# The experts' second product with tokens in the rows: 9 products of 512 columns for 12 of 384, shares applied to the outputs, and PE transposing the sum for the last stage

## The chip, the cores and the metric

One core of one Trainium2 chip. The metric is the device time of one execution in microseconds, median of several runs. PE is TensorE, DVE is VectorE, ACT is ScalarE, POOL is GpSimd, SP is the engine that issues most of the DMA transfers.

## What is computed

Three stages, one after the other on N = 1152 tokens of width 512:

```
x = banded attention(q, k, v)                       # 2 batches, 8 heads of 64, window 64
p = probs / sum(probs)                              # [N, 4], "the shares"
for e in 4 experts:                                 # F = 1024 hidden
    h = max(x @ w1[e], 0)
    out += p[:, e] * (h @ w2[e])
h = out @ w_in;  g = h * cos(h);  result = g @ w_out    # 2048 hidden, run as two halves of 1024
```

## The kernel before

Every float32 product on PE is made of three products of rounded parts: high by high, high by low, low by high (names `x_hi`, `x_lo`, `w_hi`, `w_lo`, `hp_hi`, `hp_lo`). The four experts and the two halves of the last layer are six blocks of 1024 hidden units. A block goes over three groups of TOK = 384 tokens; one group of one block is a **turn**, and a turn has FC = 8 **steps**, one for each 128 hidden units. So there are 12 expert turns (numbers 0 to 11) and 6 turns of the last layer, and 96 expert steps.

A step on PE is an up product and a down product. `up` makes 128 hidden units x 384 tokens, 12 matmuls of 384 columns (4 pieces of the input width, 3 parts each). `down` adds the step's hidden units to the turn's output. PE runs up three steps ahead of down (LAG = 3), so the order is up(s+3), down(s), up(s+4), down(s+1).

Between the two, in an expert step: DVE takes the up product out of its PSUM bank with max(.,0) times the share (`weigh`, L654; the shares lie broadcast over all partitions in `p_bc`), ACT rounds it to `hp_hi` (L493), and DVE subtracts to get `hp_lo` (L648). In the last layer ACT and DVE compute the cosine in its place (L498, L681, L683, L686, L505, L507, L694).

In an expert step the down product is laid out with output width in the rows: for each of 4 pieces of width, `w` is the stationary operand and the hidden units of 384 tokens stream through (L879: 4 x 3 matmuls of 384 columns, into the 4 banks `y_ps`). The sum `acc` is therefore width x tokens, the layout that the last layer's up product reads as its input. In the last layer the down product has the tokens in the rows: for each of 3 pieces of 128 tokens the hidden units are stationary and 512 columns of `w_out` stream (L882: 3 x 3 matmuls of 512 columns, 3 banks). At the end of a turn DVE adds the banks to `acc` (`take_outputs`, L673 and L675). After the last expert POOL rounds and subtracts `acc` into `x_hi` and `x_lo` (`next_input`, L428 and L430).

The first expert's first turn is woven into the attention: in each of its 8 steps PE has, besides up and down, the transposes of attention weights (`transpose_probs`, L827), the attention outputs (`outputs`, L843) and the scores of a later unit (`scores`, L807). The down product is cut in two there, in front of `outputs` and behind it. DVE takes the row maxima of the scores (L614) and copies the first transposed half out of PSUM (`copy_first`, L629), ACT the second half.

The order on each engine is written out by hand and kept by semaphores. The shares come in by one DMA of 72 rows of 256 bytes (L448), DVE divides (L597 to L603), and they go to a scratch area in DRAM and back by broadcasting DMAs into `p_bc`.

Of the kernel before, what the change touches and what calls it, by code (L numbers as in the profile page):

```python
# [17 lines left out]
P = 128  # L18
# [19 lines left out]
OC = TOK // P  # L38
HALVES = F2 // F1
TURN = NTOK * FC  # L40
LAG = 3
BLOCKS = E + HALVES

# [45 lines left out]
def build(nc, q, k, v, probs, weights, out):  # L89
    with ExitStack() as ctx:  # L90
# [11 lines left out]
        p_bc = sb("p_bc", [P, E, N])  # L102
# [39 lines left out]
        JP = 16  # L142
        dp_raw = part(JP, E)
        dp_sum = part(JP)
        dp_inv = part(JP)
        dp_out = part(E, JP)
# [20 lines left out]
        p_scratch = nc.dram_tensor("p_scratch", [E, N], F32, kind="Internal").ap()  # L167
# [22 lines left out]
        dp_in, dp_done, dp_stored = sem("dp_in"), sem("dp_done"), sem("dp_stored")  # L190
        p_first_tile_in, p_first_in, p_in = sem("p_first_tile_in"), sem("p_first_in"), sem("p_in")
# [13 lines left out]
        h_taken = sem("h_taken")  # L205
# [3 lines left out]
        y_taken = sem("y_taken")  # L209
        x2_hi_done = sem("x2_hi_done")  # L210
# [6 lines left out]
        C_H, C_HI, C_DOWN, C_Y = HB, HP, HP, DC  # L217
# [3 lines left out]
        def y_count(turn, c):  # L221
            if isinstance(turn, int) and turn >= MIX:
                return MIX * DC + (turn - MIX) * OC + c + 1 + C_Y
            return turn * DC + c + 1 + C_Y
# [13 lines left out]
        def _(sp):  # L238
# [36 lines left out]
            for f in range(FIRST):  # L275
# [3 lines left out]
            sp.wait_ge(dp_done, 4)  # L279
            sp.dma_start(p_scratch.rearrange("e (p j) -> p e j", j=JP),  # L280
                         dp_out[0:N // JP, :, :]).then_inc(dp_stored, 16)
# [6 lines left out]
            sp.wait_ge(dp_stored, 16)  # L288
            sp.dma_start(p_bc[:, 0, 0:TOK], p_scratch[0:1, 0:TOK].to_broadcast([P, TOK])).then_inc(p_first_tile_in, 16)
# [15 lines left out]
            sp.dma_start(p_bc[:, 0, TOK:N], p_scratch[0:1, TOK:N].to_broadcast([P, N - TOK])).then_inc(p_first_in, 16)  # L305
            load_v(8)
            load_qk(11)
            for e in range(1, E):
                load_v(8 + e)
                sp.dma_start(p_bc[:, e, :], p_scratch[e:e + 1, :].to_broadcast([P, N])).then_inc(p_in, 16)  # L310
# [18 lines left out]
        def _(pool):  # L329
# [92 lines left out]
            def next_input(t):  # L422

                pool.wait_ge(y_taken, y_count((E - 1) * NTOK + t, DC - 1))
                for c in range(DC):
                    cell = acc[:, t, c * TOK:(c + 1) * TOK]
                    at = slice(t * TOK, (t + 1) * TOK)
                    nc.gpsimd.tensor_copy(x_hi[:, c, at], cell).then_inc(x2_hi_done, 1)  # L428
                    pool.wait_ge(x2_hi_done, t * DC + c + 1)
                    last = nc.gpsimd.tensor_tensor(x_lo[:, c, at], cell, x_hi[:, c, at], ALU.subtract)  # L430
                last.then_inc(x2_lo_done, 1)

# [3 lines left out]
            for t in range(NTOK - 1):  # L436
                next_input(t)
            for f in range(FC):
                low_weights(f, E * FC + f, COS_PART)
            next_input(NTOK - 1)  # L440
# [5 lines left out]
        def _(act):  # L446
            act.sem_inc(hp_hi_done, C_HI)
            act.dma_start(dp_raw[0:N // JP, :, :],  # L448
                          probs.rearrange("(p j) e -> p j e", j=JP)).then_inc(dp_in, 16)
# [40 lines left out]
            def hidden_high(f, s):  # L490
                act.wait_ge(h_taken, s + 1 + C_H)
                act.wait_ge(down_done, s - HP + 1 + C_DOWN)
                nc.scalar.activation(hp_hi[:, f % HP, :], h_raw[:, f % HP, :], ACT.Copy).then_inc(hp_hi_done, 1)  # L493

            def cosine(f, s, late, refill=None):
# [4 lines left out]
                if late:  # L500
                    hidden_high((f - 1) % FC, s - 1)
# [7 lines left out]
            def act_turn(e, t, turn, mix_now, mix_next, last=False):  # L509
                refills = isinstance(t, int) and t == NTOK - 1 and not last  # L510
                for f in range(FC):
                    g, s = (f + LAG) % FC, turn * FC + f + LAG
                    if last and f >= FC - LAG:
                        if f == FC - LAG:
                            hidden_high(FC - 1, s - 1)
                        continue

                    refill = (f - 1, e + 1) if refills and f > 0 else None
                    if mix_now if f < FC - LAG else mix_next:
                        hidden_high(g, s)  # L520
                        if refill is not None:
                            high_weights(*refill)
                    else:
                        cosine(g, s, not (isinstance(s, int) and s == MIX * FC), refill)
                if refills:
                    high_weights(FC - 1, e + 1)
# [22 lines left out]
            for f in range(FC):  # L549
# [3 lines left out]
                if f == 0:  # L553
                    hidden_high(0, 0)
                    copy_second(m)
                    hidden_high(1, 1)
                    hidden_high(2, 2)
                    hidden_high(3, 3)
                    exponentials(m + 2, 0)
                else:  # L560
                    if f <= FIRST:
                        hidden_high(f + FIRST - 1, f + FIRST - 1)
                    elif f > FIRST + 1:
                        hidden_high((f - 1 + LAG) % FC, f - 1 + LAG)
# [8 lines left out]
            hidden_high((FC - 1 + LAG) % FC, FC - 1 + LAG)  # L573
# [9 lines left out]
            for e in range(E - 1, BLOCKS):  # L583
                with act.Fori(0, NTOK - 1) as t:
                    act_turn(e, t, e * NTOK + t, e < E, e < E)
                act_turn(e, NTOK - 1, e * NTOK + NTOK - 1, e < E, False, last=e == BLOCKS - 1)


        @block.vector
        def _(dve):  # L590
            dve.sem_inc(h_taken, C_H)
            dve.sem_inc(y_taken, C_Y)

            def shares():
                dve.wait_ge(dp_in, 16)
                rows = slice(0, N // JP)
                nc.vector.tensor_reduce(dp_sum[rows, :], dp_raw[rows, :, :], axis=AX.X, op=ALU.add).then_inc(dp_done, 1)  # L597
                dve.wait_ge(dp_done, 1)
                nc.vector.tensor_scalar_add(dp_sum[rows, :], dp_sum[rows, :], EPS).then_inc(dp_done, 1)
# [442 lines left out]
```

## Time and profile before

| | |
|---|---|
| median of 3 runs | 651.83 us (651.81 to 651.86) |
| profiled execution | 651.55 us, of which the recorded span is 649.8 us |
| PE busy | 640.1 us, 99% |
| DVE, ACT, POOL busy | 48%, 36%, 29% |

The span runs from the first to the last recorded instruction; 1.75 us of the execution's time lie outside it. The chain of work that ended last is the list of instructions that, followed back from the end, each waited for the one before; what isn't on it had time to spare. Busy time of PE is modelled from pipelined matmuls which overlap, so the distance between the starts of two matmuls, not their duration, is what one costs.

### The profile page before, as it was taken

What the parts mean: (1) busy time and instruction counts of PE and PEld (TensorE: products, weight loads), DVE (VectorE), ACT (ScalarE), POOL (GpSimd) and SP (SyncE); (2) the same over time, 40 slices, a digit from 0 to 9 for tenths busy, and PEclk for the clock granted to TensorE, in tenths of its full rate; (3) what the DMA queues carried; (4) which work ended last, traced back from release to release, by engine and by line L of the source; (5) the groups of instructions that cost most, each with busy time, mean ns of one, the idle gap of its engine ahead of it and who ended that gap; (6) DMA issues with size and microseconds to landing.
All of it is one profiled execution on the core that took longest, in us unless ns stands there. A gap on an engine that the chain in (4) does not pass through costs nothing.

```text
span 649.8 us, 11012 instructions
## 1 busy us (share of the span) xinstructions
PE 640.1 (99%) x3980; PEld 610.1 (94%) x3980; DVE 311.8 (48%) x725; ACT 234.8 (36%) x505; POOL 185.2 (29%) x246
## 2 busy tenths in 40 slices
PE   7899999999999999999999999999999999999998
PEld 6788899999999999999999999999999999999996
DVE  6676442324232324232324242325766676756664
ACT  6685411133111133111133111137455467544452
POOL 6683200154000055000056012098800059400000
PEclk8999999999999999999999999999999999999999
DMA  8858300044000034000024100023200003001011
GB/s 277 284 166 253 127 2 0 2 130 130 1 0 0 0 100 149 10 0 0 0 93 123 46 0 0 0 66 104 92 2 1 0 33 98 0 2 48 0 49 48
DMA packets 21829, 39.59 MB, mean 61 GB/s; under 512 B 2080, under 2 KB 13472, under 8 KB 21792
## 3 DMA queue, kind: packets, MB, share of 16 engines
q1 hardware_dynamic: 21708, 39.08, 18.5%
q8 instruction: 23, 0.38, 0.2%
q14 instruction: 14, 0.11, 0.1%
q10 hardware_dynamic: 84, 0.02, 0.0%
HBM read 36.72 MB, written 2.38 MB: 60 GB/s over the span
## 4 chain that ended last, share of the span: by engine, by line
PE 96%; DVE 2%; issue 1%; ACT 1%; POOL 0%; DVEq 0%
PE bank L851 45%; PE bank L879 31%; PE bank L882 15%; PE bank L843 2%; PE bank L807 1%; PE bank L827 1%; DVE arena L614 1%; PE bank L917 1%; ACT arena L457 0%; DVE arena L629 0%; DVE arena L675 0%; DVE hp_lo L648 0%; ACT x_hi L470 0%; POOL arena L389 0%; DVE arena L634 0%
## 5 line engine op out<-in xcount | busy, mean ns | idle before, releaser
L363 POOL TENSOR_TENSOR w_lo<-w_raw,w_hi 128x128 fp32r<-128x128 f32 (+2 forms) x180 | 140.5, 812 | 287.5 <-ACT w_hi L488 286.0
L851 PE MATMUL bank<-x_hi,w_hi 128*128 128x384 f32 (+1 forms) x576 | 195.0, 339 | 0.0
L851 PE MATMUL bank<-x_hi,w_lo 128*128 128x384 f32 (+1 forms) x576 | 193.2, 335 | 0.0
L851 PE MATMUL bank<-x_lo,w_hi 128*128 128x384 f32 (+1 forms) x576 | 192.8, 335 | 0.0
L493 ACT ACTIVATE hp_hi<-h_raw 128x384 fp32r<-128x384 f32 x144 | 75.3, 523 | 287.4 <-DVE h_raw L654 283.0
L654 DVE SCALAR_TENSOR_TENSOR h_raw<-bank,p_bc 128x384 f32<-128x384 f32 x96 | 53.4, 557 | 175.8 <-PE bank L851 175.0
L879 PE MATMUL bank<-hp_hi,w_hi 128*128 128x384 f32 x384 | 129.7, 338 | 0.0
L879 PE MATMUL bank<-hp_hi,w_lo 128*128 128x384 f32 x384 | 128.4, 334 | 0.0
L879 PE MATMUL bank<-hp_lo,w_hi 128*128 128x384 f32 x384 | 128.3, 334 | 0.0
L648 DVE TENSOR_TENSOR hp_lo<-h_raw,hp_hi 128x384 fp32r<-128x384 f32 x144 | 89.4, 621 | 53.7 <-ACT hp_hi L493 53.5
L851 PEld LDWEIGHTS bank<-x_hi,w_hi 128*128 128x128 f32 x576 | 108.1, 188 | 3.4 <-issue 1.0
L851 PEld LDWEIGHTS bank<-x_lo,w_hi 128*128 128x128 f32 x576 | 108.2, 188 | 1.9
L851 PEld LDWEIGHTS bank<-x_hi,w_lo 128*128 128x128 f32 x576 | 108.1, 188 | 0.0
L879 PEld LDWEIGHTS bank<-hp_hi,w_hi 128*128 128x128 f32 x384 | 72.1, 188 | 0.5
L879 PEld LDWEIGHTS bank<-hp_lo,w_hi 128*128 128x128 f32 x384 | 72.1, 188 | 0.0
L879 PEld LDWEIGHTS bank<-hp_hi,w_lo 128*128 128x128 f32 x384 | 72.0, 188 | 0.0
L882 PE MATMUL bank<-w_lo,hp_hi 128*128 128x512 f32 x144 | 56.9, 395 | 0.0
L882 PE MATMUL bank<-w_hi,hp_lo 128*128 128x512 f32 x144 | 56.8, 395 | 0.0
L882 PE MATMUL bank<-w_hi,hp_hi 128*128 128x512 f32 x144 | 56.0, 389 | 0.0
L505 ACT ACTIVATE arena<-arena 128x384 f32<-128x384 f32 x48 | 25.2, 525 | 48.1 <-DVE arena L686 48.1
L694 DVE TENSOR_TENSOR h_raw<-arena,bank 128x384 f32<-128x384 f32 x48 | 26.5, 552 | 32.5 <-ACT arena L507 32.5
L488 ACT ACTIVATE w_hi<-w_raw 128x1024 fp32r<-128x1024 f32 x40 | 41.9, 1047 | 0.1
(55 smaller groups left out, 471.4 us busy)
## 6 DMA issues: line engine op xcount, KB each, us to landing
w_raw<-in_weights SPq DMA_DIRECT2D x43, 512.0 KB, 3.5
arena<-in_q SPq DMA_DIRECT2D x12, 192.0 KB, 4.5
result<-arena SPq DMA_DIRECT2D x9, 256.0 KB, 2.1
w_raw<-in_weights SPq DMA_DIRECT2D x8, 256.0 KB, 6.3
arena<-in_k SPq DMA_DIRECT2D x8, 224.0 KB, 5.7
p_bc<-p_scratch SPq DMA_DIRECT2D x3, 576.0 KB, 5.5
arena<-in_v SPq DMA_DIRECT2D x4, 384.0 KB, 5.9
arena<-in_v SPq DMA_DIRECT2D x4, 320.0 KB, 6.4
```

The lines of the kernel that those rows point to most:

```text
L363: last = nc.gpsimd.tensor_tensor(w_lo[:, f, at:at + part], raw[:, at - begin:at - begin + part], w_hi[:, f, at:at + part], ALU.subtract)
L488: nc.scalar.activation(w_hi[:, f, :], w_raw[:, f % STAGE, :], ACT.Copy).then_inc(w_hi_done, 1)
L493: nc.scalar.activation(hp_hi[:, f % HP, :], h_raw[:, f % HP, :], ACT.Copy).then_inc(hp_hi_done, 1)
L505: nc.scalar.activation(c_abs, c_r2, ACT.Abs).then_inc(cos_abs, 1)
L614: last = nc.vector.tensor_tensor_reduce(out=s_sb[:, g % SR, t, :], in0=s_banks(m)[h][:, chunk(t)], in1=mask[:, MASK_OF[m // PAIRS][t], :], ...
L648: nc.vector.tensor_tensor(hp_lo[:, f % HP, :], h_raw[:, f % HP, :], hp_hi[:, f % HP, :], ALU.subtract).then_inc(hp_lo_done, 1)
L654: nc.vector.scalar_tensor_tensor(out=h_raw[:, f % HP, :].unsqueeze(1), in0=ps[:, 0:TOK].unsqueeze(1), scalar=0.0, in1=p_bc[:, ds1(e), toke ...
L694: nc.vector.tensor_tensor(h_raw[:, f % HP, :], c_cos, bank_h, ALU.mult).then_inc(h_taken, 1)
L843: last = nc.tensor.matmul(o_bank(m)[heads, block_of * WIN:(block_of + 1) * WIN], v_w[:, r, WINDOW_OF[t][block_of], heads], prob_t[:, h, bl ...
L851: last = nc.tensor.matmul(ps[:, 0:TOK], w[:, f, chunk(c)], x[:, c, token_cols(t)], start=c == 0 and i == 0, stop=c == DC - 1 and i == 2)
L879: product = nc.tensor.matmul(y_ps[c][:, 0:TOK], w[:, f, DM + c * P:DM + (c + 1) * P], h[:, f % HP, :], **flags)
L882: product = nc.tensor.matmul(y_ps[c][:, :], h[:, f % HP, chunk(c)], w[:, f, DM:2 * DM], **flags)
```

## The change

- `down` has the tokens in the rows in all six blocks: 3 pieces x 3 parts of 512 columns. The fourth bank, `y_ps[3]`, is free of it.
- The shares are kept with the tokens on the partitions (`p_tok`, 128 x 4 x 9), loaded by a DMA whose runs are 4 numbers (16 bytes) long, 1152 of them. The scratch area, `p_bc` and their DMAs are gone. DVE multiplies when it adds a turn's outputs (`take_shared`).
- `weigh` is gone. ACT makes `hp_hi` from the PSUM bank with Relu, and DVE makes `hp_lo` from the same bank as max(.,0) minus `hp_hi` in one instruction; the bank is free only then. In the first turn the up products alternate between two banks (`h_bank`).
- `acc` now has tokens in the rows, so PE transposes it in 9 groups of 4 transposes of 128 x 128 (`turn_input`), one behind each of steps 3, 4 and 5 of turns 10, 11 and 12; ACT rounds (`next_input_high`) and DVE subtracts (`next_input_low`) from `y_ps[3]`. POOL has no part in it.

```diff
-            def weigh(f, s, e, t, ps):
-                dve.wait_ge(up_done, s + 1)
-                nc.vector.scalar_tensor_tensor(out=h_raw[:, f % HP, :].unsqueeze(1), in0=ps[:, 0:TOK].unsqueeze(1),
-                                               scalar=0.0, in1=p_bc[:, ds1(e), token_cols(t)],
-                                               op0=ALU.max, op1=ALU.mult).then_inc(h_taken, 1)
+            def hidden_high(f, s, ps):
+                act.wait_ge(up_done, s + 1)
+                act.wait_ge(down_done, s - HP + 1 + C_DOWN)
+                nc.scalar.activation(hp_hi[:, f % HP, :], ps[:, 0:TOK], ACT.Relu).then_inc(hp_hi_done, 1)
+            def hidden_low(f, s, ps):
+                dve.wait_ge(hp_hi_done, s + 1 + C_HI)
+                nc.vector.scalar_tensor_tensor(out=hp_lo[:, f % HP, :], in0=ps[:, 0:TOK], scalar=0.0,
+                                               in1=hp_hi[:, f % HP, :], op0=ALU.max,
+                                               op1=ALU.subtract).then_inc(hp_lo_done, 1)
...
-                        if mix:
-                            product = nc.tensor.matmul(y_ps[c][:, 0:TOK], w[:, f, DM + c * P:DM + (c + 1) * P],
-                                                       h[:, f % HP, :], **flags)
-                        else:
-                            product = nc.tensor.matmul(y_ps[c][:, :], h[:, f % HP, chunk(c)], w[:, f, DM:2 * DM],
-                                                       **flags)
+                        product = nc.tensor.matmul(y_ps[c][:, :], h[:, f % HP, chunk(c)], w[:, f, DM:2 * DM],
+                                                   start=f == 0 and i == 0, stop=f == FC - 1 and i == 2)
...
+            def take_shared(e, turn, t):
+                nc.vector.tensor_copy(p_now[:, :].unsqueeze(1),
+                                      p_tok[:, ds1(e), bass.ds(t * OC, OC)]).then_inc(p_picked, 1)
+                dve.wait_ge(p_picked, turn + 1)
+                dve.wait_ge(down_done, turn * FC + FC + C_DOWN)
+                for c in range(OC):
+                    cell = acc[:, ds1(t), c * DM:(c + 1) * DM]
...
+                        nc.vector.scalar_tensor_tensor(out=cell, in0=y_ps[c][:, :].unsqueeze(1),
+                                                       scalar=p_now[:, c:c + 1], in1=cell, op0=ALU.mult,
+                                                       op1=ALU.add).then_inc(y_taken, 1)
...
+            def turn_input(k):
+                pe.wait_ge(y_taken, y_count(MIX - NTOK + k // OC, k % OC))
+                if k > 0:
+                    pe.wait_ge(x2_lo_done, k)
+                for c in range(DC):
+                    at = k % OC * DM + c * P
+                    last = nc.tensor.transpose(y_ps[3][:, chunk(c)], acc[:, k // OC, at:at + P], ident[:, :])
+                last.then_inc(x2_turned, 1)
...
-                down_cells(f, True, (0, 1), 0)
+                down_cells(f, (0,), 0)
...
-                    down_cells(f, True, (2, 3), 0).then_inc(down_done, 1)
+                    down_cells(f, (1, 2), 0).then_inc(down_done, 1)
...
-            act.dma_start(dp_raw[0:N // JP, :, :],
-                          probs.rearrange("(p j) e -> p j e", j=JP)).then_inc(dp_in, 16)
+            act.dma_start(dp_raw, probs.rearrange("(k p) e -> p k e", p=P)).then_inc(dp_in, 16)
```

On PE, a down product inside an expert turn, before (L879 is `down_cells`, L851 the up product behind it):

```order
1451 L879 MATMUL bank<-hp_hi,w_hi 128x384 [waits hp_lo_done]
1452 L879 MATMUL bank<-hp_lo,w_hi 128x384
1453 L879 MATMUL bank<-hp_hi,w_lo 128x384
1454 L879 MATMUL bank<-hp_hi,w_hi 128x384
1455 L879 MATMUL bank<-hp_lo,w_hi 128x384
1456 L879 MATMUL bank<-hp_hi,w_lo 128x384
1457 L879 MATMUL bank<-hp_hi,w_hi 128x384
1458 L879 MATMUL bank<-hp_lo,w_hi 128x384
1459 L879 MATMUL bank<-hp_hi,w_lo 128x384
1460 L879 MATMUL bank<-hp_hi,w_hi 128x384
1461 L879 MATMUL bank<-hp_lo,w_hi 128x384
1462 L879 MATMUL bank<-hp_hi,w_lo 128x384
```

The down product at such a place after the change, in one of the nine steps that have transposes behind them (L892 is `down_cells`, L911 `turn_input`, L865 the up product):

```order
1456 L892 MATMUL bank<-w_hi,hp_hi 128x512 [waits hp_lo_done]
1457 L892 MATMUL bank<-w_hi,hp_lo 128x512
1458 L892 MATMUL bank<-w_lo,hp_hi 128x512
1459 L892 MATMUL bank<-w_hi,hp_hi 128x512
1460 L892 MATMUL bank<-w_hi,hp_lo 128x512
1461 L892 MATMUL bank<-w_lo,hp_hi 128x512
1462 L892 MATMUL bank<-w_hi,hp_hi 128x512
1463 L892 MATMUL bank<-w_hi,hp_lo 128x512
1464 L892 MATMUL bank<-w_lo,hp_hi 128x512
1465 L911 MATMUL bank<-ident,arena 128x128 [waits x2_lo_done,y_taken]
1466 L911 MATMUL bank<-ident,arena 128x128 x3
1467 L865 MATMUL bank<-x_hi,w_hi 128x384 [waits hp_lo_done,w_lo_done]
```

Twelve matmuls of 384 columns became nine of 512, and four transposes stand ahead of the next up product.

On DVE, in the second step of the woven turn, behind the last of six maxima (`arena` holds the attention's tiles; the ISA rows are the maxima), before:

```order
148 L614 ISA arena<-bank,mask 128x128
149 L614 ISA arena 128x1
150 L648 TENSOR_TENSOR hp_lo<-h_raw,hp_hi 128x384 [waits hp_hi_done]
151 L629 COPY arena<-bank 128x384 [waits p_transposed]
152 L623 TENSOR_SCALAR arena<-arena 128x3 [waits exped]
153 L625 RECIPROCAL arena<-arena 128x3 [waits summed]
154 L623 TENSOR_SCALAR arena<-arena 128x3 [waits exped]
155 L625 RECIPROCAL arena<-arena 128x3 [waits summed]
156 L654 SCALAR_TENSOR_TENSOR h_raw<-bank,p_bc 128x384 [waits hp_hi_done,up_done,hp_lo_done]
157 L643 TENSOR_TENSOR x_lo<-bank,x_hi 128x384 [waits x_hi_done]
```

The same place after:

```order
141 L613 ISA arena<-bank,mask 128x128
142 L613 ISA arena 128x1
143 L647 SCALAR_TENSOR_TENSOR hp_lo<-bank,hp_hi 128x384 [waits hp_hi_done]
144 L628 COPY arena<-bank 128x384 [waits p_transposed]
145 L622 TENSOR_SCALAR arena<-arena 128x3 [waits exped]
146 L624 RECIPROCAL arena<-arena 128x3 [waits summed]
147 L622 TENSOR_SCALAR arena<-arena 128x3 [waits exped]
148 L624 RECIPROCAL arena<-arena 128x3 [waits summed]
149 L642 TENSOR_TENSOR x_lo<-bank,x_hi 128x384 [waits x_hi_done]
```

The subtraction now reads PSUM and one SBUF tile, and `weigh` is gone from behind it.

## Rows read from the trace of the kernel before

**Rows 1.** The page: busy time of PE and the clock granted to it, in 40 slices.

```profile
PE 640.1 (99%) x3980; PEld 610.1 (94%) x3980; DVE 311.8 (48%) x725; ACT 234.8 (36%) x505; POOL 185.2 (29%) x246
...
PEclk8999999999999999999999999999999999999999
```

**Rows 2.** Groups of instructions, by form: busy us, mean ns | idle before.

```profile
L879 PE MATMUL bank<-hp_hi,w_hi 128*128 128x384 f32 x384 | 129.7, 338 | 0.0
...
L882 PE MATMUL bank<-w_hi,hp_lo 128*128 128x512 f32 x144 | 56.8, 395 | 0.0
```

**Rows 3.** The chain in order of time: start us, us, what.

```profile
88.07 2.08 PE bank L879 x12
...
449.99 2.08 PE bank L879 x12
452.07 2.08 PE bank L851 x12
454.15 2.08 PE bank L882 x9
456.23 2.10 PE bank L851 x12
...
634.17 2.08 PE bank L882 x9
```

**Rows 4.** DVE in order of time, first cosine step: start us, us, instruction.

```profile
442.23 0.65 DVE L681 TENSOR_SCALAR arena<-arena 128x384 f32<-128x384 f32 x1 [2.88 <-ACT arena L498]
```

**Rows 5.** PE in order of time, the woven turn.

```profile
73.83 0.33 PE L851 MATMUL bank<-x_hi,w_hi 128*128 128x384 f32 x1
...
74.87 0.49 PE L827 MATMUL bank<-ident,arena 128*128 128x128 f32 x3
...
76.24 0.49 PE L827 MATMUL bank<-ident,arena 128*128 128x128 f32 x3
```

**Rows 6.** Groups by form: copies, subtractions, additions and PE's old transposes.

```profile
L648 DVE TENSOR_TENSOR hp_lo<-h_raw,hp_hi 128x384 fp32r<-128x384 f32 x144 | 89.4, 621 | 53.7 <-ACT hp_hi L493 53.5
...
L827 PE MATMUL bank<-ident,arena 128*128 128x128 f32 x72 | 12.5, 287 | 2.7 <-DVE arena L629 1.9 <-POOL arena L389 0.8
...
L478 ACT ACTIVATE w_hi<-w_raw 128x512 fp32r<-128x512 f32 x4 | 2.5, 620 | 0.0
...
L675 DVE TENSOR_TENSOR arena<-bank,arena 128x512 f32<-128x512 f32 x3 | 2.0, 691 | 1.8 <-PE bank L882 1.8
```

**Rows 7.** One cosine step in order of time, PE, ACT and DVE.

```profile
562.67 0.33 PE L851 MATMUL bank<-x_hi,w_lo 128*128 x1
...
565.69 0.62 ACT L507 ACTIVATE arena<-arena,half_pi 128x384 f32<-128x384 f32 x1
...
566.43 0.56 DVE L694 TENSOR_TENSOR h_raw<-arena,bank 128x384 f32<-128x384 f32 x1 [0.86 <-ACT arena L507]
```

**Rows 8.** The chain in order of time, the woven turn.

```profile
41.98 0.94 DVE hp_lo L648
...
49.46 0.87 DVE hp_lo L648
```

**Rows 9.** PE in order of time, two places in the woven turn.

```profile
43.54 0.52 PE L827 MATMUL bank<-ident,arena 128*128 128x128 f32 x3 [0.33 <-DVE arena L629]
...
63.61 0.34 PE L879 MATMUL bank<-hp_hi,w_lo 128*128 128x384 f32 x1
63.99 0.89 PE L807 MATMUL bank<-arena 64*64 64x128 f32 x24
```

**Rows 10.** The first 7 us in order of time, DVE and PE.

```profile
3.04 0.22 DVE L597 TENSOR_REDUCE arena<-arena 72x16 f32<-72x64 f32 x1 [1.85 <-DMA arena<-in_probs]
...
3.81 0.28 DVE L603 TENSOR_TENSOR arena<-arena 72x64 f32<-72x64 f32 x1
...
6.04 0.29 DVE L614 CUSTOM_DVE_ANT_0 arena<-bank,mask 128x128 f32<-128x128 f32 x1 [1.96 <-PE bank L807]
...
6.26 0.89 PE L807 MATMUL bank<-arena 64*64 64x128 f32 x24 [0.41 <-DMA arena<-in_k]
```

More of the change, by code:

```diff
@@ L141, in build @@
         row_inv = part(PR, CT)
[L142 to L146, printed above, removed]
+        dp_raw = part(TILES, E)
+        dp_sum = part(TILES)
+        dp_inv = part(TILES)
         bank = [ctx.enter_context(nc.psum_tensor(f"bank{i}", [P, 512], F32)) for i in range(8)]
@@ L165, in o_bank, with h_bank @@
             return bank[0] if m < AHEAD else pt_ps
-        p_scratch = nc.dram_tensor("p_scratch", [E, N], F32, kind="Internal").ap()
+        def h_bank(s):
+            if s < FIRST:
+                return y_ps[s]
+            return y_ps[3] if s % 2 else bank[0]
         ident_done = sem("ident_done")
@@ L420, in _ @@
                     low_second(i + 2)
[L422 to L431, printed above, removed]
             with pool.Fori(1, E) as e:
@@ L658, in share, with next_input_low @@
-            def share(f, s, e, t):
-                weigh(f, s, e, t, h_ps[f % HB])
-                hidden_low(f, s)
-            def take_outputs(e, turn, t, mix, last=False):
-                if isinstance(e, int) and e == E:
-                    dve.wait_ge(x2_lo_done, t + 1)
+            def next_input_low(k):
+                dve.wait_ge(x2_hi_done, k + 1)
+                cell = (slice(None), slice(None), slice(k * P, (k + 1) * P))
+                nc.vector.tensor_tensor(x_lo[cell], y_ps[3][:, :].rearrange("p (c n) -> p c n", c=DC), x_hi[cell],
+                                        ALU.subtract).then_inc(x2_lo_done, 1)
@@ L665, in take_outputs @@
+            def take_outputs(e, turn, t, last=False):
+                if e == E:
+                    dve.wait_ge(x2_lo_done, (t + 1) * OC)
                 if not last:
                     dve.wait_ge(down_done, turn * FC + FC + C_DOWN)
[L667 removed]
+                for c in range(OC):
                     if last:
                         dve.wait_ge(result_done, c + 1)
[L670 to L675 removed]
@@ L677, in times_cosine @@
-            def times_cosine(f, s, late, take=None):
+                    cell = acc[:, ds1(t), c * DM:(c + 1) * DM]
+                    if e == E:
+                        nc.vector.tensor_copy(cell, y_ps[c][:, :].unsqueeze(1)).then_inc(y_taken, 1)
+                    else:
+                        nc.vector.tensor_tensor(cell, y_ps[c][:, :].unsqueeze(1), cell, ALU.add).then_inc(y_taken, 1)
+            def times_cosine(f, s, late, take=None, which=()):
                 n = s - MIX * FC
```

249 lines of the change are left out of this document (121 added, 128 removed).

## The prediction

> **What bounds the kernel now.** I read the page's busy times and granted clock first. PE is busy 99% of the span and holds 0.9 or more of its clock in every slice but the first [rows 1]: this is the upper of its two levels, 2.4 GHz. Then the chain that ended last, in order of time: from the down product at 88.07 us to the end it is PE and nothing else, in pieces of 2.08 or 2.10 us that follow each other without a gap [rows 3]. So behind 88 us only PE's own work counts, and what DVE, ACT, POOL or the DMAs are spared there is worth nothing. Ahead of 88 us, where the attention is woven in, DVE stands in the chain, and there a shorter DVE can pay.
>
> **The change, part by part.**
>
> *The down product itself.* The groups of instructions tempt to a large gain: a 384-column matmul has a mean of 338 ns, a 512-column one 395 ns [rows 2], so 12 of the one against 9 of the other would be 4.06 against 3.56 us, 0.50 us a step, 48 us over 96 steps. But these are durations of overlapping instructions. The chain gives what they cost back to back: 12 of 384 columns take 2.08 us, 9 of 512 also 2.08 us [rows 3]. Both stream 4608 columns, 173 and 231 ns a matmul, 0.451 ns a column either way. I take 0 us.
>
> The Trainium skill, "TensorE: Matmul & The Clock Gate", section "Wait — 56ns, not 53.3ns?", speaks for a small gain here: it gives a fixed 2.5 ns for each warm matmul on top of its columns. By it, three matmuls less in each of 96 steps would save an estimated 0.7 us. The row disagrees: what 384 columns take above 160 ns (384 over 2.4 GHz) is 13 ns, and 512 above 213 ns it is 18 ns, so the excess grows with the columns and nothing of it is fixed.
>
> *The pair of up and down.* One thing does differ. Between the 384-column downs at 88.07 and 449.99 lie 87 steps, 361.92 / 87 = 4.160 us a step. Between the 512-column downs at 454.15 and 634.17 lie 43 steps, 180.02 / 43 = 4.187 us [rows 3]. The up product behind a 512-column down takes 2.10 us, not 2.08. It isn't the cosine work that does it: that begins on DVE at 442.23 [rows 4], and the up product at 452.07 still takes 2.08 [rows 3]; the first slow one, at 456.23, is the first behind a 512-column down. So each step of turns 1 to 11, 88 of them, becomes 0.027 us longer: **+2.35 us**. Bounds: 0 if it were something else of the last layer, 2.6 if the 8 woven steps have it too.
>
> *The transposes.* 36 of 128 columns, all new on PE, where nothing can hide them. In the woven turn, 12 up matmuls with one group of 3 transposes among them take 76.24 − 73.83 = 2.41 us [rows 5] against 2.08: a group of 3 costs 0.33 us, 0.11 a transpose with the changeovers. A group of 4 is then 0.44 us, nine groups **+3.95 us**. Bounds: 3.5 (one changeover less in a group) and 5.0.
>
> *Waits of the transposes.* Group k waits for `y_taken` of a turn that ended at least three steps ago, and for the `x_lo` of group k−1, one step (4.19 + 0.44 us) ago. In between, ACT rounds 128x512, near 0.62 us, and DVE subtracts, near 0.69 us [rows 6], both behind their own step's work. In a cosine step ACT gets to it behind the sine, which ended at 566.31, and DVE behind the multiplication, at 566.99; the step's up product ended its 12 matmuls at 562.84 [rows 7]. So `x_lo` is there some 4.8 us behind the up product (4.15 and 0.69), and the next group comes 2.08 + 0.44 + 2.10 + 2.08 = 6.7 us behind it. Queued behind that wait are all later matmuls, so it would cost one for one if it came; I take 0, bound 1 us. The last layer's first up products need `x_lo` of groups that end a turn earlier: 0. POOL is rid of `next_input`, which had time to spare: 0.
>
> *DVE and ACT in the expert turns.* `weigh` goes, `hp_lo` comes from PSUM by the same kind of instruction as `weigh` (0.56 us, as for the multiplication out of PSUM [rows 7], for the old mean of 0.62 [rows 6]), and each turn ends with three multiply-adds of 128x512, near 0.69 us each, and a small copy. PE needs the first bank 2.08 us after the turn's end and each later one 0.69 us on; DVE delivers in step with that, ahead by over 1 us. Covered by the up product: 0. The longer hold of the up banks (until `hp_lo`, not `weigh`) has four banks of slack: 0. The broadcasts leave a queue on which nobody on the chain waits: 0.
>
> *The woven turn.* Three terms.
> - In steps 1 and 2, DVE's chain is maxima, `hp_lo`, `copy_first`, and PE's next transposes wait for it. `hp_lo` takes 0.94 and 0.87 us there [rows 8] against a mean of 0.62 [rows 6]; PE stood idle for it, 0.33 us on record at the first place [rows 9]. The form that reads PSUM takes 0.56 us [rows 7], some 0.48 of it in the chain if the next instruction overlaps it as elsewhere: 0.94 + 0.87 − 2 x 0.48 = **−0.85 us**. Bounds of the gain: 0.4, if it meets whatever slows the old form, and 0.85, since both stalls are then closed.
> - The down product was halved around `outputs`, 1.04 us on each side; now it is one third ahead, 0.69, and two behind, 1.39. In step 4 the first part stands in front of `scores`, which waits for DVE's maxima, 0.2 us already (63.61 to 63.99, less 0.17 for the matmul) [rows 9]. It will wait 0.35 more and the second part is 0.35 longer: **+0.35 us**. In the other steps the thinner cover (0.35 us) is over ACT's copy of 0.5 us and just holds; bound 0.1 each for five steps.
> - The start. The DMA of the shares goes from 72 rows to 1152 runs of 16 bytes, in front of which DVE stands: all maxima are queued behind the division of the shares. Before, it landed at 3.04, the division took 1.05 us, and the first maximum came at 6.04, when the scores were there [rows 10]. So the landing may slip 1.9 us for nothing. The same DMA engines bring q and k, and the second scores already wait 0.41 us for k until 6.26 [rows 10]. I take **+0.3 us** for that; bounds 0 and 3.5 (a landing near 8.5 us).
>
> The sum: 2.35 + 3.95 − 0.85 + 0.35 + 0.3 = +6.1 us on the profiled execution's 651.55 (649.8 of span and 1.75 around it), 657.65; the median of the runs lies 0.28 higher, so 657.9. I say **657.9 us**, 0.9% slower. This likeliest case alone: 656.0 to 659.6.
>
> **The rivals.**
> - *The shares come late.* If the small runs take turns with the large ones of q and k one by one on each DMA engine, the landing slips beyond 5 us and DVE's whole queue, hence PE at the start, by up to 3 us more: 659.5 to 661.5. For it: 16 times as many descriptors. Against: 3 us is much for 18 KB, and there are 1.9 us of slack. 0.10.
> - *A new wait in the change of layers or the woven turn.* A group of transposes arrives before `x_lo`, or `outputs` before ACT's copy: 1 to 4 us, 659 to 662. The margins above speak against it. 0.06.
> - *The 2.10 us belongs to the last layer,* and the woven turn loses nothing for its 0.85: 651.83 + 3.95 − 0.85 = 654.9, with its spread 653.9 to 655.6. Against it is the up product at 452.07. 0.08.
> - *Fewer matmuls are cheaper after all.* One mechanism: a matmul has a fixed cost which the chain's pace hides at 384 columns. It decides from 6.1 / 288 = 21 ns a matmul (288 matmuls go away); at 30 ns it would give 657.9 − 8.6 = 649.3, at the 167 ns that the durations suggest (0.50 us for three) 610. The equal 2.08 us say it is 0. Faster 0.03, within 0.2% 0.02.
> - *Transposes cost their duration.* 36 x 287 ns [rows 6] = 10.3 in place of 3.95: 664. The 0.33 us for three speak against it. 0.01. The Trainium skill, "TensorE: Matmul & The Clock Gate", section "Part 4: PE-mode transpose", gives about 275 ns for one in a kernel; the trace's mean duration agrees with that, its distance from start to start doesn't.
>
> **How the numbers follow.** The forecast has 0.70; with the rivals at 0.10, 0.06, 0.08, 0.05 and 0.01 that makes 1. The range must reach into the late shares above and into the 654.9 case below: 654.5 to 661.2 leaves out some 0.15. About 0.2%, 1.3 us, is what a measurement of this kernel can tell from no change. Slower by more than that are all but the case of fixed cost: slower 0.95, same 0.02, faster 0.03.
>
> **What the profile after would show.** Right: the chain from 88 us on has downs of 9 at 2.08 and ups of 12 at 2.10 us in the expert turns, 4.187 us a step; nine groups of four transposes, each adding 0.44 us, with no idle time of PE ahead of them; DVE busy well below 48%; the pauses ahead of 43.5 and 50.9 us gone, the one at 63.6 grown to over 0.5 us. Wrong: a step of 4.16 us or below it; transposes with a releaser; a first maximum much after 6.1 us; POOL, ACT or DVE in the chain behind 88 us.

## The result, and the profile after

| | before | after |
|---|---|---|
| median of the runs side by side | 651.82 us (4 runs, 651.36 to 651.86) | 655.23 us (4 runs, 654.78 to 655.44) |
| profiled execution, its span | 651.55, 649.8 us | 654.78, 653.0 us |
| DVE, POOL busy | 48%, 29% | 40%, 25% |

The ratio is 1.0051, 95% interval 1.0038 to 1.0063: 3.4 us slower, where I had forecast 6.1. The direction and the larger term were right; what I had priced at 2.35 us came to less than nothing.

The page of the kernel after: busy times and the granted clock.

```profile
PE 642.1 (98%) x3728; PEld 576.5 (88%) x3728; DVE 259.6 (40%) x638; ACT 235.7 (36%) x514; POOL 163.6 (25%) x222
...
PEclk9999999999999999999999999999999999999999
```

PE issued 252 matmuls fewer than in [rows 1] (288 gone, 36 transposes new), and its busy time rose by 2 us. The clock stayed at its upper level. Groups by form, after (busy us, mean ns | idle before):

```profile
L892 PE MATMUL bank<-w_hi,hp_hi 128*128 128x512 f32 x432 | 170.9, 396 | 0.1
L911 PE MATMUL bank<-ident,arena 128*128 128x128 f32 x36 | 5.4, 272 | 0.0
L647 DVE SCALAR_TENSOR_TENSOR hp_lo<-bank,hp_hi 128x384 fp32r<-128x384 f32 x96 | 53.3, 557 | 264.4 <-ACT hp_hi L476 264.4
```

The durations of L892 answer to L882's in [rows 2] and say nothing of the pace. The transposes (L911) have no idle time before them and no releaser. The chain after in order of time (start us, us, what); L865 is the up product, L892 the down product, L821 and L857 the scores and outputs of the woven turn:

```profile
39.59 0.82 PE bank L821 x24
...
53.62 0.82 PE bank L821 x24
...
60.63 0.86 PE bank L821 x24
...
65.78 0.87 PE bank L857 x24
...
85.25 2.11 PE bank L865 x12
87.35 2.06 PE bank L892 x9
...
399.85 2.06 PE bank L892 x9
401.92 0.44 PE bank L911 x4
...
406.51 0.44 PE bank L911 x4
...
454.47 2.11 PE bank L865 x12
456.58 0.05 issue
456.63 2.33 PE bank L892 x9
458.96 1.06 PE bank L865 x6
...
639.41 2.11 PE bank L865 x12
641.51 6.88 PE bank L892 x30
```

The same chain of before, at places not shown yet (L807 are the scores of the woven turn and L843 its outputs; step 4 begins with the scores at 61.61):

```profile
39.75 0.86 PE bank L807 x24
...
54.63 0.82 PE bank L807 x24
...
61.61 0.82 PE bank L807 x24
...
66.41 0.87 PE bank L843 x24
...
85.75 2.32 PE bank L851 x12
...
636.26 2.10 PE bank L851 x12
638.36 6.86 PE bank L882 x30
```

From these rows the 3.15 us between the two last pieces (641.51 and 638.36) can be taken apart; what stands behind them differs by less than 0.1 us.

- Woven turn: the first down product behind it starts at 87.35 instead of 88.07 [rows 3]: **−0.72**.
- Expert steps: (399.85 − 87.35) / 75 = 4.167 us instead of 4.160, in 88 steps: **+0.6**. The down product takes 2.06 us where I expected 2.08, the up product 2.11.
- Transposes: with a group, a step takes 406.51 − 401.92 = 4.59 to 4.60 us, 0.43 more than without. Nine of them: **+3.85**.
- The first down product of the last layer pauses: 0.05 us ahead of 456.63, and 2.33 us instead of 2.06: **+0.3**.
- Last layer, whose code on PE is unchanged: before, 43 steps from 456.23 [rows 3] to 636.26 are 4.187 us each; after, from the up product that follows the pause at 458.96 to the one at 639.41, 180.45 us with three groups of transposes (1.3 us) among them: 4.166 each, **−0.9**.

Together +3.1. The last item is the odd one: the same instructions on PE in the same order became faster.

### The profile page after: what moved, and what is told of

It reads as the page before. It is cut to its first block, busy times and chain, and to the rows that moved or that the text cites. A ratio compares the mean times of both kernels' runs of the same rounds, so it can differ in the third digit from the quotient of the medians.

```text
span 653.0 us, 10127 instructions
## 1 busy us (share of the span) xinstructions
PE 642.1 (98%) x3728; PEld 576.5 (88%) x3728; DVE 259.6 (40%) x638; ACT 235.7 (36%) x514; POOL 163.6 (25%) x222
## 4 chain that ended last, share of the span: by engine, by line
PE 96%; DVE 2%; issue 1%; ACT 1%; DMA 1%; POOL 0%; SPq 0%; DVEq 0%
PE bank L865 46%; PE bank L892 45%; PE bank L857 2%; PE bank L821 1%; PE bank L841 1%; DVE arena L613 1%; PE bank L911 1%; DMA arena<-in_k 1%; ACT arena L440 0%; DVE arena L690 0%; DVE arena L628 0%; ACT x_hi L453 0%; POOL arena L387 0%; DVE arena L633 0%; SPq L248 0%
## 5 line engine op out<-in xcount | busy, mean ns | idle before, releaser
L361 POOL TENSOR_TENSOR w_lo<-w_raw,w_hi 128x128 fp32r<-128x128 f32 (+2 forms) x180 | 138.1, 798 | 370.5 <-ACT w_hi L471 368.4
L865 PE MATMUL bank<-x_hi,w_hi 128*128 128x384 f32 (+1 forms) x576 | 196.9, 342 | 0.0
L865 PE MATMUL bank<-x_hi,w_lo 128*128 128x384 f32 (+1 forms) x576 | 194.7, 338 | 0.0
L865 PE MATMUL bank<-x_lo,w_hi 128*128 128x384 f32 (+1 forms) x576 | 193.5, 336 | 0.0
L892 PE MATMUL bank<-w_hi,hp_hi 128*128 128x512 f32 x432 | 170.9, 396 | 0.1
L892 PE MATMUL bank<-w_hi,hp_lo 128*128 128x512 f32 x432 | 170.3, 394 | 0.0
L892 PE MATMUL bank<-w_lo,hp_hi 128*128 128x512 f32 x432 | 168.1, 389 | 0.0
L647 DVE SCALAR_TENSOR_TENSOR hp_lo<-bank,hp_hi 128x384 fp32r<-128x384 f32 x96 | 53.3, 557 | 264.4 <-ACT hp_hi L476 264.4
L476 ACT ACTIVATE hp_hi<-bank 128x384 fp32r<-128x384 f32 x96 | 46.9, 491 | 278.1 <-PE bank L865 275.8
L865 PEld LDWEIGHTS bank<-x_hi,w_hi 128*128 128x128 f32 x576 | 108.3, 188 | 7.1 <-issue 1.0
L865 PEld LDWEIGHTS bank<-x_lo,w_hi 128*128 128x128 f32 x576 | 108.3, 188 | 4.9
L865 PEld LDWEIGHTS bank<-x_hi,w_lo 128*128 128x128 f32 x576 | 108.0, 188 | 0.0
L892 PEld LDWEIGHTS bank<-w_lo,hp_hi 128*128 128x128 f32 x432 | 81.1, 188 | 18.1
L892 PEld LDWEIGHTS bank<-w_hi,hp_hi 128*128 128x128 f32 x432 | 81.0, 188 | 13.3 <-issue 0.3
L892 PEld LDWEIGHTS bank<-w_hi,hp_lo 128*128 128x128 f32 x432 | 81.3, 188 | 10.6
L440 ACT ACTIVATE arena<-arena 128x128 f32<-128x128 f32 x72 | 27.9, 392 | 12.4 <-PE bank L841 6.5
L501 ACT ACTIVATE arena<-arena,half_pi 128x384 f32<-128x384 f32 x48 | 29.6, 617 | 1.5
```

The lines of the kernel that those rows point to most:

```text
L361: last = nc.gpsimd.tensor_tensor(w_lo[:, f, at:at + part], raw[:, at - begin:at - begin + part], w_hi[:, f, at:at + part], ALU.subtract)
L440: last = nc.scalar.activation(prob[:, g % PR, t, :], s_sb[:, g % SR, t, :], ACT.Exp, bias=neg_max[:, g % PR, t:t + 1], scale=-1.0, accum_o ...
L476: nc.scalar.activation(hp_hi[:, f % HP, :], ps[:, 0:TOK], ACT.Relu).then_inc(hp_hi_done, 1)
L501: nc.scalar.activation(c_cos, c_abs, ACT.Sin, bias=half_pi[:, 0:1], scale=-1.0).then_inc(cos_done, 1)
L647: nc.vector.scalar_tensor_tensor(out=hp_lo[:, f % HP, :], in0=ps[:, 0:TOK], scalar=0.0, in1=hp_hi[:, f % HP, :], op0=ALU.max, op1=ALU.subt ...
L865: last = nc.tensor.matmul(ps[:, 0:TOK], w[:, f, chunk(c)], x[:, c, token_cols(t)], start=c == 0 and i == 0, stop=c == DC - 1 and i == 2)
```

## The experiments

Line numbers are shifted a little where an edit adds or removes lines. Those called "the kernel before" or "after" differ from it only by the edit shown. Beside each one the kernel before was run again: 651.75 to 651.79 us.

### Why the pace changed: the place of the tiles

What could reach the last layer's pace was memory. The change removes `p_bc` (18,432 bytes a partition), which lies ahead of `hp_hi`, and puts `p_tok` and `p_now` there. In the program as laid out, with tiles padded to 32 bytes, the tiles of the hidden units moved by 192 bytes against the weights' tiles, modulo 512. All distances below are `hp_hi` less `w_hi` in bytes, counted modulo 512 (the remainder when multiples of 512 are taken off): 0 before, 192 after.

**A gap of the old size.** An unused tile behind `p_now`; because of the padding the distance becomes 64 and not the old 0.

```diff
+        gap = sb("gap", [P, E * N - E * TILES - OC])
         hp_hi = sb("hp_hi", [P, HP, TOK], F32R)
```

> The changed kernel with an unused tile of 18 KB a partition where the shares' tile stood before, so that every tile behind it has its old address. The nine 512-column matmuls of a down product took 2.081 us in the last layer before and take 2.061 us now, with the same code. Theory A, the address of the hidden units' tiles sets it: 2.081 us again in all 136 steps behind the woven turn, 655.2 + 2.7 = 657.9 us. Theory B, it comes from the rest of the change or from the run: 2.061 us and 655.2 us.

Measured: 659.59 us, ratio 1.0121 (1.0105 to 1.0136). An unused tile costs 4.4 us on the kernel after. Its chain:

```profile
301.58 2.10 PE bank L893 x9
...
305.78 2.10 PE bank L893 x9
```

4.200 us a step, in the experts and in the last layer. Place matters, then, though this isn't the old place.

**The kernel before with `p_bc` allocated last.** The hidden units' tiles move by 18,432 bytes, 36 x 512; the distance stays 0.

```diff
-        p_bc = sb("p_bc", [P, E, N])
         hp_hi = sb("hp_hi", [P, HP, TOK], F32R)
...
+        p_bc = sb("p_bc", [P, E, N])
```

> The kernel before, with the tile of the broadcast shares allocated behind all others instead of in the middle; nothing else. Theory A, address: the last layer's down products fall from 2.081 to 2.061 us, 48 x 0.02 = 1.0 us less, 650.9 us. Theory B, not the address: 651.8 us, 2.081 us.

Measured: 651.75 us, ratio 0.9999 (0.9990 to 1.0008), 4.160 and 4.187 us a step as before. So a move of the hidden units' tiles by 18 KB does nothing by itself.

**The kernel after with `hp_hi` at an address divisible by 512** (distance 384), against the theory that the address itself counts:

```diff
+        gap = sb("gap", [P, 48])
         hp_hi = sb("hp_hi", [P, HP, TOK], F32R)
```

> The changed kernel with an unused 192 bytes a partition in front of the tiles of the hidden units, so that these begin at an address divisible by 512. So far the pairs of down and up took 2.081 + 2.106 us with these tiles at 128 above a multiple of 256 (both places), 2.061 + 2.106 at 64 above, 2.100 + 2.100 at 192 above. Theory A, the address below 256 bytes sets the pace of PE: another pair of values at 0, I guess at or below 2.061 + 2.106, 655.2 us or up to 2 us less. Theory B, it isn't the address but what lies beside it: 2.061 + 2.106.

Measured: 659.56 us, ratio 1.0118 (1.0102 to 1.0133), 2.09 us for a down and 2.11 for an up product, 4.200 us a step. My guess under theory A, 655.2 us or less, was wrong by over 4 us.

**All tiles moved together by 384 bytes**, distances unchanged. It is built on the kernel before with `copy_first` moved (below, 650.69 us), so it is to be compared with that one.

```diff
+        gap = sb("gap", [P, 96])
         w_hi = sb("w_hi", [P, FC, 2 * DM], F32R)
```

> The kernel before, with the copy ahead of the subtraction (650.7 us) and with an unused 384 bytes a partition in front of all tiles, so that every operand of a matmul begins at an address divisible by 512; all began at 128 above a multiple of 256 before. Theory A, absolute address: the pace of the expert steps leaves 4.160 us (either way), the total moves by several us. Theory D, only the distance between the tiles of w and x and those of the hidden units counts, and that is unchanged: 4.160 and 4.187 us, 650.7 us.

Measured: 650.48 us, ratio 0.9982 (0.9973 to 0.9991), 4.160 and 4.187 us a step. Here the absolute address of every operand moved and no pace changed. The last layer's step also differs from the 4.200 us of the run before, though `hp_hi` begins at a multiple of 512 in both. So the absolute address alone doesn't set the pace.

**The kernel after at distance 0**, with 320 unused bytes. This is the kernel that my prediction was in fact about.

```diff
+        gap = sb("gap", [P, 80])
         hp_hi = sb("hp_hi", [P, HP, TOK], F32R)
```

> The changed kernel with an unused 320 bytes a partition in front of the hidden units' tiles, which brings their distance from w and x to a multiple of 512, as it was in the kernel before. Theory, only that distance sets the pace of alternating 512- and 384-column products: 2.081 + 2.106 us a step as in the last layer before, in all 136 steps behind the woven turn, 655.2 + 136 x 0.020 = 657.9 us, the forecast's figure. Rival, the value belongs to this kernel's other tiles too (shares, sum): any other pair of values.

Measured: 657.45 us, ratio 1.0088 (1.0074 to 1.0103). Its chain has the 2.08 and 2.10 us of the last layer before [rows 3]:

```profile
351.31 2.08 PE bank L893 x9
353.39 2.10 PE bank L866 x12
...
363.87 2.08 PE bank L893 x9
```

(363.87 − 351.31) / 3 = 4.187 us a step, the pace I had forecast.

**The kernel after at distance 224**, with 32 bytes (`gap` of 8 numbers at the same line).

> The changed kernel with an unused 32 bytes a partition in front of the hidden units' tiles: distance 224 (mod 512), 32 more than now (192, 4.167 us a step). Known are 0 (4.187), 64 (4.200), 384 (4.200). If the pace goes smoothly with the distance: 4.17 to 4.18 us, 655.7 to 657 us. If it goes by steps of 64 bytes: 4.167 us, 655.2 us.

Measured: 660.68 us, ratio 1.0138 (1.0122 to 1.0155), slower than either guess. The pace is a third one, from 32 bytes:

```profile
352.63 2.10 PE bank L893 x9
354.73 2.11 PE bank L866 x12
...
365.25 2.10 PE bank L893 x9
```

(365.25 − 352.63) / 3 = 4.207 us a step.

**The kernel before at the distance of after, 192**, again with `copy_first` moved. Its last layer should become fast.

```diff
+        gap = sb("gap", [P, 48])
         hp_hi = sb("hp_hi", [P, HP, TOK], F32R)
```

> The kernel before with the copy ahead of the subtraction (650.7 us) and with an unused 192 bytes a partition in front of the hidden units' tiles: the distance of the changed kernel. Theory: the last layer's steps fall from 4.187 to 4.167 us, 1.0 us in all, while the expert steps, all of 384 columns, stay at 4.160: 649.7 us, the best of all. Rival: the expert steps are sensitive to the distance too and leave 4.160.

Measured: 650.57 us, ratio 0.9981 (0.9972 to 0.9990). The chain, an expert step (L877 is its down product) and one of the last layer (L880):

```profile
351.63 2.09 PE bank L849 x12
353.72 2.08 PE bank L877 x12
...
364.13 2.09 PE bank L849 x12
...
541.22 2.06 PE bank L880 x9
...
553.72 2.06 PE bank L880 x9
```

The last layer went from 4.187 to (553.72 − 541.22) / 3 = 4.167 us, the pace of the kernel after: that part held. The time did not fall, because the expert steps went from 4.160 to (364.13 − 351.63) / 3 = 4.167, which I hadn't expected: 88 x 0.007 = 0.6 us back.

**The same 320 bytes, but behind `hp_lo`.** All kernels with a gap so far had also moved `h_raw` and the arena, which ACT and DVE read and write. Here only those move.

```diff
         hp_lo = sb("hp_lo", [P, HP, TOK], F32R)
+        gap = sb("gap", [P, 80])
         h_raw = sb("h_raw", [P, HP, TOK])
```

> The changed kernel with 320 unused bytes a partition behind hp_lo instead of in front of hp_hi: the hidden units' tiles PE reads stay 192 bytes (mod 512) from the weights, while h_raw, the small tiles and the arena, where the outputs and the attention's tiles lie, move by 320, as in the kernel with distance 0. Theory (PE's pace goes with the place of its own two operands, weights against hidden units): nothing changes, downs of 2.061 and ups of 2.106 us, 4.167 a step, 655.2 us within 0.6. Rival (it is the tiles that ACT and DVE read and write, which moved along in all the kernels with a gap): 4.187 a step, as with the gap in front, 657.4 us. If it gives another pace than either, both sets of tiles have a part.

Measured: 655.21 us, ratio 1.0056 (1.0040 to 1.0073), against 655.23 for the kernel after.

```profile
352.23 2.11 PE bank L866 x12
354.34 2.06 PE bank L893 x9
```

2.11 and 2.06 as without a gap: 4.167 us. So it is the place of `hp_hi` and `hp_lo`, not that of `h_raw` and the arena.

### Width or roles

In the last layer before, the down product is both wider (512) and has its roles exchanged (hidden units stationary). This kernel keeps the roles and makes it 12 matmuls of 384 columns; it leaves out the last quarter of the output's columns.

```diff
-                            product = nc.tensor.matmul(y_ps[c][:, :], h[:, f % HP, chunk(c)], w[:, f, DM:2 * DM],
-                                                       **flags)
+                            if c == OC - 1:
...
+                                nc.tensor.matmul(y_ps[3][:, 0:TOK], h[:, f % HP, chunk(c)], w[:, f, DM:DM + TOK],
+                                                 **flags)
+                            product = nc.tensor.matmul(y_ps[c][:, 0:TOK], h[:, f % HP, chunk(c)],
+                                                       w[:, f, DM:DM + TOK], **flags)
```

> The kernel before, where in the last layer's down product the hidden units stay stationary and w streams, but 384 columns of it in 12 matmuls in place of 512 in 9; it leaves out the last quarter of the output's columns. An up product takes 2.080 us behind a 12 x 384 down product of the expert form and 2.106 us behind a 9 x 512 one. Theory W, the width of the matmuls in front makes the difference: 2.080 us here, last layer 48 x 0.026 = 1.2 us shorter, 650.6 us. Theory R, the roles make it (hidden units stationary, w streaming): 2.106 us stays, 651.8 us.

Measured: 650.64 us, ratio 0.9981 (0.9972 to 0.9991), 1.15 us faster. In the chain of its last layer L852 is the up product, L888 and L886 the down product:

```profile
556.74 2.08 PE bank L852 x12
558.82 1.04 PE bank L888 x6
...
560.90 2.08 PE bank L852 x12
```

The step is 560.90 − 556.74 = 4.16 us, and 43 steps at 0.027 us are the 1.15. So at distance 0 the roles cost nothing at a width of 384 columns; what costs is the down product as 9 matmuls of 512 between products of 384. A down product of 512 columns in the old roles wasn't run. The down product took 560.90 − 558.82 = 2.08 us in 12 pieces, the same as in 9.

### The transposes

The kernel after without `turn_input` and what ACT and DVE do behind it. It leaves the last layer's input out.

```diff
-                    if inputs and f in TURNS:
-                        turn_input((t - 1) % NTOK * OC + TURNS.index(f))
...
-                    if inputs and f in TURNS:
-                        next_input_high((t - 1) % NTOK * OC + TURNS.index(f))
```

> The changed kernel without the 36 transposes of the sum and without the rounding and subtraction behind them; it leaves the last layer's input out (the last layer then multiplies the attention's output). Forecast's price, nine groups at 0.44 us less the 0.02 us that the next up product gains back: 655.2 - 3.8 = 651.4 us. Rival, the copies of the transposed sum also made ACT and DVE late where the last layer takes over (0.4 us of pause near 456 us): then that pause goes too, 651.0 us.

Measured: 651.36 us, ratio 0.9992 (0.9983 to 1.0001). The transposes cost 655.23 − 651.36 = 3.9 us, 0.43 a group. Its first down product of the last layer still takes 2.28 us, so most of the pause there isn't theirs.

### The woven turn

**The kernel before with `copy_first` ahead of `hidden_low` on DVE**, in all steps and not in one alone: another way to the gain that I had given to the new `hp_lo`.

```diff
-                    if f == FIRST:
-                        copy_first(m)
+                    copy_first(m)
...
-                    if f != FIRST:
-                        copy_first(m)
```

> The kernel before, with DVE's copy of the first transposed half put ahead of the subtraction that makes the low part of the hidden units, in steps 1 to 3 and 6 and 7 of the woven turn (step 4 has that order already); nothing of the change. Theory, the woven turn's gain in the changed kernel is only that this subtraction no longer stands 0.9 us long in front of the copy: two pauses of PE close, 651.8 - 0.85 = 651.0 us, and the down product at 88.1 us starts near 87.2. Rival, the gain needs the shorter DVE work as a whole: 651.5 to 651.8 us.

Measured: 650.69 us, ratio 0.9981 (0.9972 to 0.9990), 1.1 us faster than the kernel before and 4.5 faster than the one after. That is 0.3 us better than the theory: the down product behind the woven turn starts at 86.88, not near 87.2, and from the scores at 39.65 to those at 53.51 PE takes 1.02 us less than before (39.75 to 54.63), where I had put 0.85. The chain at the first place of [rows 8] has no gap on PE, and DVE isn't in it (L824 is `transpose_probs`); at the second it is the same.

```profile
43.11 0.33 PE bank L824 x3
43.44 1.05 PE bank L876 x6
```

**The kernel after, mended in two places.** Two thirds of the down product ahead of `outputs` and one third behind, to undo the loss in step 4; and at the end of turn 11 DVE takes the outputs before the cosine step's `hp_lo`, to close the pause at 456.58.

```diff
-                down_cells(f, (0,), 0)
+                if f == 0:
+                    pe.wait_ge(hp_lo_done, 2)
+                down_cells(f, (0, 1), 0)
...
-                    down_cells(f, (1, 2), 0).then_inc(down_done, 1)
+                    down_cells(f, (2,), 0).then_inc(down_done, 1)
...
-                if late:
-                    hidden_low_cos((f - 1) % FC, s - 1)
...
+                if late:
+                    hidden_low_cos((f - 1) % FC, s - 1)
```

> The changed kernel with two edits of order, each with a place of its own in the trace. First, in the woven turn two thirds of the down product stand in front of the attention outputs and one third behind, not one and two: the 0.35 us that step 4 lost should come back (a pause of 0.79 us from start to start at 62.2 us falls to 0.4 or less). Second, at the end of the last expert turn DVE takes the outputs before it makes the low part of the hidden units: the pause of 0.39 us at 456.2 should go. Together 0.35 + 0.3 us: 654.6 us. Rival: each wait only moves to the next releaser, 655.2 us.

Measured: 654.88 us, ratio 1.0045 (1.0032 to 1.0059), 0.35 us less than the kernel after. The chain at the end of the woven turn and in the change of layers:

```profile
83.04 0.87 PE bank L857 x24
...
83.93 0.50 ACT x_hi L453
...
84.46 0.57 DVE x_lo L642
...
87.43 2.06 PE bank L892 x9
...
454.55 2.11 PE bank L865 x12
456.65 2.06 PE bank L892 x9
```

The pause at 456 is gone, which is the whole gain. The split gained nothing: the down product of turn 1 starts at 87.43 instead of 87.35. With less of the down product behind `outputs`, PE now reaches the next up product before ACT and DVE have made `x_lo`. What step 4 gave back went to another waiter: of the expected 0.65 us only the seam's 0.3 came, and of the two theories the rival held for the first edit.

## Why the prediction was right, and where it wasn't

- **The down product itself, 0.** Right. At distance 0 the same place of the program, the last layer's down product, takes 2.08 us as 9 x 512 [rows 3] and as 12 x 384 columns. The Trainium skill, "TensorE: Matmul & The Clock Gate", section "Wait — 56ns, not 53.3ns?", has a fixed 2.5 ns for each warm matmul; by it the three matmuls more would take an estimated 7.5 ns a product. It doesn't show: averaged over 34 steps of the last layer (470 to 610 us), from start to start, 9 x 512 take 2.082 us and 12 x 384 take 2.080. But a change of distance moves the 9 x 512 by more (2.06 to 2.10), so these two layouts can't rule out a cost of that size, and the prediction's "nothing of it is fixed" was said too firmly.
- **The pair of up and down, +2.35.** This is the term that was mis-sized. I took the 4.187 us of the last layer before as the price of alternating 384 and 512 columns. The width was the right cause (at distance 0), and the kernel after at distance 0 has it: 4.187 us and 657.45 us, where I had forecast 657.9. But the price also hangs on where the hidden units lie against the weights, and the change moves them by putting `p_tok` and `p_now` ahead of them in place of `p_bc`. It came to +0.6 in the expert turns and −0.9 in the last layer, −0.3 for +2.35. Neither my bounds (0 and 2.6) nor a rival had the last layer in them: I had taken code that isn't edited as untouched. The rival that gives 654.9 had nearly the measured time for a wrong reason: it held that the 2.10 us belongs to the last layer. And 655.23 us lies below what I gave the likeliest case by itself (656.0 to 659.6); the whole range, 654.5 to 661.2, holds it only because it had been drawn down for that rival. That part was luck.
- **The transposes, +3.95.** Right: 3.9 by the run without them, 3.85 by the chain. Their duration of 272 ns a piece would have made 9.8.
- **Their waits, 0.** Right; no releaser.
- **DVE and ACT in the expert turns, 0.** Right but for one place. The first down product of the last layer waits 0.3 us. DVE there has a cosine step and the turn's end at once (DVE of the kernel after, in order of time):

```profile
454.54 0.82 DVE L653 TENSOR_TENSOR hp_lo<-h_raw,hp_hi 128x384 fp32r<-128x384 f32 x1
455.28 0.42 DVE L664 COPY p_now<-p_tok 128x3 f32<-128x3 f32 x1
455.74 2.07 DVE L674 SCALAR_TENSOR_TENSOR arena<-bank,p_now,arena 128x512 f32<-128x512 f32 x3
```

  On PE, the last up matmul ahead of that down product (PE in order of time):

```profile
456.24 0.34 PE L865 MATMUL bank<-x_hi,w_lo 128*128 128x384 f32 x1
```

  The down product could have begun 0.17 us behind it, at 456.41. The first of the three multiply-adds began at 455.74; they start 0.69 us apart and one takes 0.75 us by its group, so the bank it reads came free only at 456.49. I had worked out the margin in an expert turn (over 1 us) and not where two kinds of turn meet. Taking the outputs first closed it, which shows that it was this order.
- **The woven turn**, term by term:
  - The pauses ahead of 43.5 and 50.9 us are gone, as forecast, and at the forecast's price: from the scores at 39.75 to those at 54.63 the kernel before takes 14.88 us, the one after 53.62 − 39.59 = 14.03, −0.85.
  - Step 4 from its first scores to its outputs took 66.41 − 61.61 = 4.80 us before and takes 65.78 − 60.63 = 5.15 after: +0.35, as forecast. Its pause ahead of the second scores grew as foreseen: from start to start 62.23 to 63.02, 0.56 us more than the 0.23 of a matmul.
  - The start: at the scores of 39.59 and 39.75 the kernel after is 0.16 us ahead, where I expected a loss of 0.3; but this start moves by more than that between executions (39.59 to 40.19 in the eight profiled kernels with the change), so no gain or loss of it is shown.
  - Steps 5 to 7 take 0.13 us more in all (a whole step 5.95 us, not 5.88), within the bound of 0.1 each.
  - The last up product takes 2.11 instead of 2.32 us, which I had not foreseen. It is the other side of the new split: before, `x_lo` was done at 85.64 and the up product began at 85.69, right behind it; after, two thirds of the down product stand behind `outputs`, `x_lo` was done at 84.78 and the up product began at 85.08 without a pause. In the mended kernel, with one third behind, it takes 2.35 again.
  - Together −0.16 − 0.85 + 0.03 (step 3) + 0.35 + 0.13 − 0.22 = −0.72. So −0.7 for −0.2: the pauses and step 4 right, the start not as forecast, and +0.13 and −0.22 that were not in the sum.

The start of the kernel after, DVE in order of time:

```profile
4.17 0.19 DVE L597 TENSOR_REDUCE arena<-arena 128x9 f32<-128x36 f32 x1 [3.08 <-DMA arena<-in_probs]
...
5.88 0.29 DVE L613 CUSTOM_DVE_ANT_0 arena<-bank,mask 128x128 f32<-128x128 f32 x1 [0.81 <-PE bank L821]
```

DVE began on the shares 1.1 us later than at 3.04 [rows 10], inside the 1.9 us of slack, and the first maximum waited for PE's scores and not for them. The rival of late shares fell here.

The sum as it was: −0.3 for the pace, +3.9, +0.3, −0.7: +3.2 us on the profiled execution, for 3.23 measured (654.78 − 651.55).

**What stays open.** Why the distance matters isn't shown. Five distances of the kernel after gave 4.187 (0), 4.200 (64), 4.167 (192), 4.207 (224) and 4.200 us (384) a step; no rule that I can read from five points. They would fit a count modulo 256 as well (0, 64, 192, 224 and 128), so the 512 is how I counted and not a finding. Nor was a distance at which 384 and 512 columns alternate at 4.160 found, or looked for beyond these. That it is the place against the weights, rather than against the inputs `x_hi` and `x_lo`, wasn't separated either: those kept their distance to the weights in every kernel.

## What to carry to other kernels

Where PE is the whole chain, its pace hangs in hundredths of a microsecond on where its operands lie. A tile of 32 unused bytes in front of them moved the time by 0.8% here (655.2 to 660.7 us), and a change that adds or removes a tile moves code that it doesn't touch (the last layer, 0.9 us); pin the layout, or compare the change at more than one layout, before a difference of that size is put down to the change. Read a pace from the distance between starts at the same width and neighbours, and work out the margins at the seam between two kinds of turn, not only inside each. And a wait that a large change would cure may be had for less: here moving one copy on DVE gave 1.1 us, and the kernel before with that alone (650.7 us) beats the whole change. The two layouts of it that were tried, 650.5 and 650.6 us, can't be told from it.

## What the runs showed of the hardware

- Matmuls of a chain without any wait cost 4.160 to 4.207 us for the same 9216 columns, by the widths (384 with 384, or 384 with 512) and the distance between tiles. It isn't a matter of wide against narrow alone: at distance 192, 12 x 384 and 12 x 384 take 2.09 and 2.08 us, at distance 0 both 2.08.
- The subtraction that reads two tiles in SBUF (L648) took 1.02 and 0.95 us at 41.90 and 49.37 in the kernel before, where the form that reads PSUM and one SBUF tile (L647) took 0.55 at the same places after. In both kernels POOL was at work on `w_lo` (L363, L361) then. Where POOL stood idle (56.78, 64.23, 73.79 and 79.67), the old form took 0.55 too. With `copy_first` moved it still takes 0.95 us at 42.58, again beside POOL, but nothing waits for it. One at 35.50 took 0.57 beside POOL, and no run kept POOL away, so that POOL slows it is likely and not shown.
- DVE could begin on the shares at 4.07 to 4.30 us in the eight profiled kernels that load them in 1152 runs of 16 bytes, and at 2.87 to 3.07 in the six with 72 rows of 256 bytes: 1.1 us later for the same 18 KB, while q and k were under way.
